# Decayed linear attention in front of two gated layers: the attention's blocks cut from 128 to 64 tokens, its products on quarters of the array

## What is computed

```python
def _attn_ref(q, k, v, alpha):            # (4, 8, 768, 48) each
    B, H, S, D = q.shape
    state = np.zeros((B, H, D, D)); y = np.zeros_like(q)
    for t in range(S):
        state = alpha[:, :, t, :, None] * state + np.einsum('bhd,bhe->bhde', k[:, :, t], v[:, :, t])
        y[:, :, t] = np.einsum('bhd,bhde->bhe', q[:, :, t], state)
    return y

def reference(**kwargs):
    x = attention output as (3072 tokens, 384)
    x = (sigmoid(x @ w_gate) * (x @ w_val)) @ moe_w_out              # 384 -> 1536 -> 384
    return np.maximum(np.maximum(x @ w1, x @ w2), x @ w3) @ w_out    # 384 -> 768 -> 384
...
```

## Time and profile before

| | |
|---|---|
| median of 3 runs | 860.12 us (859.79 to 860.45) |
| the profiled execution, its own time | 859.93 us |
| its span, first to last instruction | 857.9 us |
| PE busy | 851.0 us, 99% |
| DVE busy | 364.2 us, 42% |
| ACT busy | 279.2 us, 33% |
| POOL busy | 75.9 us, 9% |
| chain of work that ended last | PE 97%, DVE 2% |
| mean granted TensorE clock | 0.999 |

### The profile page before, as it was taken

How to read it: one execution, slowest core, us unless ns; L and a number is a source line. 1 busy time by engine, 2 the same in 40 slices (tenths; PEclk the granted TensorE clock), 3 DMA queues, 4 the chain that set the end, 5 groups by cost and what they waited for, 6 DMA issues and landing times.

```text
span 857.9 us, 14194 instructions
## 1 busy us (share of the span) xinstructions
PE 851.0 (99%) x5653; PEld 790.4 (92%) x5653; DVE 364.2 (42%) x677; ACT 279.2 (33%) x520; POOL 75.9 (9%) x68
## 2 busy tenths in 40 slices
PE   8999999999999999999999999999999999999998
PEld 8899999999999999999999999988888888888887
DVE  8776554544454354374265232322323232232321
ACT  4555343333333333333333334421213122131312
POOL 1000111111021021021011004400000000000000
PEclk9999999999999999999999999999999999999999
DMA  7440210210210210201111023100100101010001
GB/s 282 171 169 3 99 47 2 100 47 2 99 47 2 99 47 2 87 17 44 49 51 47 7 74 112 37 1 1 37 1 1 37 0 37 0 37 0 20 17 38
DMA packets 14449, 42.14 MB, mean 49 GB/s; under 512 B 1984, under 2 KB 5952, under 8 KB 14400
## 3 DMA queue, kind: packets, MB, share of 16 engines
q1 hardware_dynamic: 14336, 41.38, 13.5%
q10 hardware_dynamic: 64, 0.05, 0.0%
HBM read 35.52 MB, written 4.72 MB: 47 GB/s over the span
## 4 chain that ended last, share of the span: by engine, by line
PE 97%; DVE 2%; issue 0%; ACT 0%; DMA 0%; ACTq 0%; DVEq 0%
PE ps_gv L915 35%; PE ps_out L940 18%; PE ps_gv L921 17%; PE ps_out L1034 6%; PE ps_sc L915 6%; PE ps_sc L921 3%; PE ps_pair L903 3%; PE ps_sc L866 2%; PE ps_pair L1034 2%; PE ps_pair L850 1%; PE ps_pair L899 1%; PE ps_sc L876 1%; DVE decay L629 0%; DVE rdec L641 0%; DMA inbuf<-att_in 0%
## 5 line engine op out<-in xcount | busy, mean ns | idle before, releaser
L915 PE MATMUL ps_gv<-x_hi,w_hi 128*128 128x384 f32 (+1 forms) x792 | 279.6, 353 | 1.1 <-ACT x_hi L404 1.1
L915 PE MATMUL ps_gv<-x_hi,w_lo 128*128 128x384 f32 (+1 forms) x792 | 277.1, 350 | 0.0
L921 PE MATMUL ps_gv<-x_lo,w_hi 128*128 128x384 f32 (+1 forms) x792 | 234.8, 350 | 0.0
L915 PEld LDWEIGHTS ps_gv<-x_hi,w_hi 128*128 128x128 f32 x792 | 148.7, 188 | 9.3 <-ACT w_hi L404 1.3
L915 PEld LDWEIGHTS ps_gv<-x_hi,w_lo 128*128 128x128 f32 x792 | 148.9, 188 | 7.5
L921 PEld LDWEIGHTS ps_gv<-x_lo,w_hi 128*128 128x128 f32 x792 | 146.0, 188 | 9.4
L719 DVE TENSOR_TENSOR h_sb<-act_sb,ps_gv 128x384 f32<-128x384 f32 x96 | 53.0, 552 | 164.1 <-PE ps_gv L921 163.5
L404 ACT ACTIVATE h_hi<-h_sb 128x384 fp32r<-128x384 f32 x96 | 50.4, 525 | 150.7 <-DVE h_sb L719 150.6
L450 ACT ACTIVATE act_sb<-ps_gv 128x384 f32<-128x384 f32 x96 | 47.2, 491 | 131.2 <-PE ps_gv L921 131.2
L816 DVE TENSOR_TENSOR probs<-probs,ps_gv 128x512 f32<-128x512 f32 x36 | 24.8, 689 | 137.9 <-PE ps_gv L921 137.9
L677 DVE TENSOR_TENSOR h_lo<-h_sb,h_hi 128x384 fp32r<-128x384 f32 x96 | 54.1, 564 | 52.0 <-ACT h_hi L404 52.0
(11 more groups left out here) (123 smaller groups left out, 973.7 us busy)
## 6 DMA issues: line engine op xcount, KB each, us to landing
inbuf<-att_in SPq DMA_DIRECT2D x23, 704.0 KB, 4.7
mid<-w SPq DMA_DIRECT2D x12, 576.0 KB, 8.4
inbuf<-att_in SPq DMA_DIRECT2D x23, 256.0 KB, 3.0
inbuf<-w SPq DMA_DIRECT2D x6, 768.0 KB, 4.3
out<-inbuf SPq DMA_DIRECT2D x5, 768.0 KB, 3.5
x_raw<-x_raw SPq DMA_DIRECT2D x46, 24.0 KB, 1.9
out<-inbuf SPq DMA_DIRECT2D x4, 192.0 KB, 2.0
mid<-att_in SPq DMA_DIRECT2D x1, 704.0 KB, 9.0
```

The source lines that it names most:

```text
L915: mm(bank, w_at(half, f, c + k * P, total=total), x_hi[:, k, 0:w], start=(k == 0 and half == 0), stop=False)
L921: return mm(bank, w_at(0, f, c + k * P, total=total), x_lo[:, k, 0:w], start=False, stop=(k == KT - 1))
```

## The change

Each chunk of 128 tokens is computed as two blocks of `SB` = 64 (`SUBS` = 2).
- `scans` and `recips` make eight scans of 64 and of 63 elements a chunk instead of four of 128 and of 127; a block's decay starts anew.
- `scores` computes only the two diagonal blocks: 16 matmuls, each 48 rows by 64 weight columns with 64 moving columns, on four quarters of the array. `masked` then handles 256 instead of 512 elements a partition, twice. `probs` has two buffers, by the chunk's parity.
- `outer` makes one outer product for each block: 16 matmuls with 64 rows, into two PSUM banks (`ps_sc`, `ps_sc_odd`). It comes ahead of `attend`: after the value product of f = 2, 5, 8.
- `new_state` makes two steps of two VectorE operations instead of one step of two, on three state buffers; it moves from the block after `attend` to f = 2, 5, 8, behind `h_rest`.
- `attend` uses for each block the state ahead of it: 16 matmuls with 64 moving columns (8 where the chunk opens a batch, none before). The values are 16 matmuls of 64 rows and 64 moving columns in two groups of 8; ahead of the second group PE waits for its own semaphore `y_same`, which the last of the first group sets.
- `attend` now waits for this chunk's own new states; in the prologue for the first of the two. `new_state` waits for the `attend` of the chunk before (`y_done`).
- the number of `unused` matmuls in the prologue is changed, and w1's block 5 no longer waits for chunk 1's `probs`, which have moved out of its slot.

```diff
+SB = 64
+SUBS = CH // SB
...
-        probs = sb("probs", [P, H, CH])
-        state = sb("state", [P, 2, PAIRS, D])
+        probs = sb("probs", [P, 2, H, SB])
+        state = sb("state", [P, 3, PAIRS, D])
...
                 for p in range(PAIRS):
-                    nc.vector.tensor_tensor_scan(decay[0:PR, par, p, :], att(buf(Cs), ALPHA)[:, p, :],
-                                                 zero[0:PR, :].broadcast_to([PR, CH]), 1.0, ALU.mult, ALU.add).then_inc(scan_done, 1)
+                    for s in range(SUBS):
+                        nc.vector.tensor_tensor_scan(decay[0:PR, par, p, sub(s)], att(buf(Cs), ALPHA)[:, p, sub(s)],
+                                                     zero[0:PR, :].broadcast_to([PR, SB]), 1.0,
+                                                     ALU.mult, ALU.add).then_inc(scan_done, 1)
...
             def new_state(Cs, i):
 
-                C, cur, new = Cs + 6 * i, Cs % 2, (Cs + 1) % 2
+                C = Cs + 6 * i
                 dve.wait_ge(u_done, C + 1)
...
+                if not (isinstance(i, int) and Cs == 0):
+                    dve.wait_ge(y_done, C)
+                for s in range(SUBS):
+                    next_state(Cs, i, s)
...
-                    done = (C0 + c - 1, i) if att_next and f % 3 == 0 and c > 0 else None
...
-                    if done:
-                        new_state(*done)
+                    if att and f % 3 == 2:
+                        new_state(*att)
...
-                    for r, bank in zip(HALVES, score_banks(Cs, i)):
-                        ins = mm(bank[:, p * CH:(p + 1) * CH], att(buf(Cs), K, r)[:, p, :],
-                                 att(buf(Cs), Q, r)[:, p, :], start=True, stop=True)
+                    for s in range(SUBS):
+                        for r, bank in zip(HALVES, score_banks(Cs, i)):
+                            ins = mm(bank[sub(s), p * SB:(p + 1) * SB], att(buf(Cs), K, r)[:, p, sub(s)],
+                                     att(buf(Cs), Q, r)[:, p, sub(s)], start=True, stop=True)
...
                 for p in range(PAIRS):
-                    for n, r in enumerate(HALVES):
-                        ins = mm(outer_bank(Cs, i)[r, p * D:(p + 1) * D],
-                                 khs[:, p * PR + r.start:p * PR + r.stop],
-                                 v_cols(buf(Cs), (2 * p + n) * D, D), start=True, stop=True)
+                    for s in range(SUBS):
+                        for n, r in enumerate(HALVES):
+                            ins = mm(outer_bank(Cs, i, s)[r, p * D:(p + 1) * D],
+                                     khs[sub(s), p * PR + r.start:p * PR + r.stop],
+                                     v_cols(buf(Cs), (2 * p + n) * D, D)[sub(s), :], start=True, stop=True)
...
+            def value(Cs, i, p, n, s):
+                return mm(y_slot(Cs, i, p, n, s), v_cols(buf(Cs), (2 * p + n) * D, D)[sub(s), :],
+                          probs[sub(s), Cs % 2, PAIRS * n + p, :], start=False, stop=True, skip_group_check=True)
...
+                for s in range(1 if first else 0, SUBS):
                     for p in range(PAIRS):
                         for n, r in enumerate(HALVES):
...
                 for p in range(PAIRS):
                     for n in range(2):
+                        ins = value(Cs, i, p, n, n)
+                ins.then_inc(y_same, 1)
+                pe.wait_ge(y_same, C + 1)
+                for p in range(PAIRS):
+                    for n in range(2):
+                        ins = value(Cs, i, p, n, 1 - n)
                 ins.then_inc(y_done, 1)
...
+                    if att_next and f in (2, 5, 8):
+                        outer(C0 + (f - 2) // 3, i)
                     if att_next and f in (3, 6, 9):
                         attend(C0 + (f - 3) // 3, i)
-                        outer(C0 + (f - 3) // 3, i)
```

More of the change, by code:

```diff
@@ L183, in score_banks, with sub, ends @@
             return ps_sc, ps_sc_odd
[L185 to L189, removed]
+        def sub(s):
+            return slice(s * SB, (s + 1) * SB)
+        def ends(x):
+            return x.rearrange("q a (s t) -> q a s t", s=SUBS)[:, :, :, SB - 1]
         def arrived(eng, sems, Cs, i):
@@ L413, in khs_copy @@
                 act.wait_ge(u_done, C)
-                copy(khs[:, :], u_bank(Cs, i)[:, 0:PAIRS * PR]).then_inc(khs_done, 1)
+                copy(khs[:, :], tr_bank(Cs, i)[:, 0:PAIRS * PR]).then_inc(khs_done, 1)
             def y_copy(Cs, i):
@@ L648, in masked @@
                 if half == 0 and not (isinstance(i, int) and Cs < 2):
[L649 to L652, removed]
+                    dve.wait_ge(y_done, C - 1)
@@ new lines, in new_state, with next_state @@
+                for s in range(SUBS):
+                    next_state(Cs, i, s)
+            def next_state(Cs, i, s):
+                j = Cs * SUBS + s
+                old, new = state[0:PR, j % 3], state[0:PR, (j + 1) % 3]
+                u = outer_bank(Cs, i, s)[0:PR, :].rearrange("p (a e) -> p a e", a=PAIRS)
+                end = decay[0:PR, Cs % 2, :, (s + 1) * SB - 1:(s + 1) * SB].broadcast_to([PR, PAIRS, D])
+                if j % (2 * CPT * SUBS) == 0:
+                    nc.vector.tensor_tensor(new, u, end, ALU.mult).then_inc(state_done, 1)
+                else:
+                    dve.wait_ge(state_done, j + 6 * SUBS * i)
+                    nc.vector.tensor_tensor(stmp[0:PR], u, old, ALU.add).then_inc(stmp_done, 1)
+                    later = j - j // (2 * CPT * SUBS) - 1 + (6 * SUBS - 1) * i
@@ L667, in new_state @@
                     dve.wait_ge(stmp_done, later + 1)
-                    nc.vector.tensor_tensor(state[0:PR, new], stmp[0:PR], end, ALU.mult).then_inc(state_done, 1)
+                    nc.vector.tensor_tensor(new, stmp[0:PR], end, ALU.mult).then_inc(state_done, 1)
             def x_rest(k, n, src, w=TOK):
@@ L891, in attend @@
                     pe.wait_ge(y_evac, C)
[L892 to L896, removed]
+                    pe.wait_ge(state_done, (C + 1) * SUBS)
+                else:
+                    if Cs == 2:
+                        pe.wait_ge(y_evac, 1)
+                    pe.wait_ge(state_done, C * SUBS + 1)
+                for s in range(1 if first else 0, SUBS):
                     for p in range(PAIRS):
                         for n, r in enumerate(HALVES):
-                            mm(y_slot(Cs, i, p, n), state[r, par, p, :], att(buf(Cs), Q, r)[:, p, :],
-                               start=(p < 2), stop=False, skip_group_check=True)
+                            mm(y_slot(Cs, i, p, n, s), state[r, (Cs * SUBS + s) % 3, p, :],
+                               att(buf(Cs), Q, r)[:, p, sub(s)], start=(p < 2 and s == (1 if first else 0)),
+                               stop=False, skip_group_check=True)
                 for p in range(PAIRS):
                     for n in range(2):
-                        ins = mm(y_slot(Cs, i, p, n), v_cols(buf(Cs), (2 * p + n) * D, D),
-                                 probs_of(Cs, i)[:, PAIRS * n + p, :],
-                                 start=(first and p < 2), stop=True, skip_group_check=True)
+                        ins = value(Cs, i, p, n, n)
[4 more added lines that the diff above has]
+                        ins = value(Cs, i, p, n, 1 - n)
                 ins.then_inc(y_done, 1)
@@ L989, in general, with unused @@
                     ins.then_inc(gen_sum, 1)
-            def unused(n, left, right):
+            def unused(n, bank, left, right):
                 for _ in range(n):
-                    mm(ps_out[:, 2, 0:CH], left, right, start=True, stop=True)
+                    mm(ps_out[:, bank, 0:right.shape[-1]], left, right, start=True, stop=True)
             zeros = state[:, 0, :, :].rearrange("p a e -> p (a e)")
             pe.wait_ge(state_zero, 1)
-            unused(15, zeros[:, 0:P], zeros[:, D:D + CH])
+            unused(12, 2, zeros[:, 0:P], zeros)
             scores(0, 0)
@@ L1007, in _ @@
             attend(0, 0)
+            unused(4, 0, ident, ident)
             outer(1, 0)
-            unused(10, ident, mask)
+            unused(7, 0, ident, ident)
             scores(2, 0)
```

87 lines of the change are left out of this document (46 added, 41 removed).

## The result

The changed kernel takes **863.1 us** (median of 7 runs, 861.54 to 863.53) against 860.43 (859.79 to 860.72) of the kernel before in the same session: ratio 1.0029, interval 1.002 to 1.0039. It is slower by 0.3%, where 856.9 and "faster" were forecast, and lies 0.1 us above the range.

A forecast was written before the change was run, and what follows sets the result against it. PE's instruction stream was taken as the bound (busy 851.0 of 857.9 us). Layer 1 -6.7 and prologue +3.5 sum to -3.2: 856.7 on the profiled run, 856.9 us as median; range 851.8 to 863.

The forecast's parts named there:

- the prologue's chain: Prologue: scores of chunk 2 start once its k is scaled, 2.3 us later; copy of y and first product +3.5 us.
- The `unused` matmuls fill PE's waits and don't shift this: Prologue: the filler matmuls on PE add nothing to the +3.5 us delay of the first product.
- Rival 2: Prologue takes the gain: half scans cost nearly a whole, or longer chain, +6 and more; `y_same` dearer; 860 to 862, chance 0.2.
- Its clause on longer waits at half clock: Prologue: longer PE waits ahead of the first product could cost a stretch at half clock; part of the 0.2 chance.
- the groups of four at 0.058: PE inside layer 1: a group of four passes with 64 columns takes 0.058 us, interpolated between 0.046 and 0.108.
- `attend` 1.55 (1.57): PE inside layer 1: state and value matmuls with the wait on `y_same` sum to 1.57 us a chunk.
- a batch-opening chunk at 0 (-0.48 + 0.46): Layer 1, three chunks: scores save 0.48 us, outer and attend add 0.46, since half a state product is new.
- layer 1 -6.76 (-6.7): PE over layer 1's 21 chunks: scores -10.1, outer and attend +2.0 and +1.4, together -6.7 us.
- h's delay covered: VectorE inside layer 1: h comes 1.0 us late but costs nothing, with 4.7 us of PE work as cover.
- forecast +0.7: Prologue, VectorE: half scans, forward and backward, take 0.7 us more a chunk, between 0 and +3.0.
- Rival 1: PE in layer 1: too many passes, averaging no less than 0.023 us; +24 us, 881 us; chance 0.13 in full or part.
- The test that the prediction set: Prologue: a first product after 33 us would show the forecast wrong; near 31.2 would show it right.

The follow-up runs named there:

- the first experiment: The changed kernel, but outer(1) in the prologue waits for chunk 0's masks alone, not chunk 1's; 857.56 us, ratio 0.9971.
- the fifth experiment: The kernel of the first experiment with chunk 1's two states made ahead of chunk 2's masks on VectorE; 857.6 us, ratio 0.9965.
- second experiment: The changed kernel with 22 instead of 4 unused matmuls between attend(0) and outer(1) in the prologue; 860.83 us, ratio 1.0008.

## Why the prediction was wrong

**The failed step** is the prologue's chain: "PE's scores of chunk 2 start when chunk 2's k is scaled", and its sum +3.5. It followed the scores to their own releaser and not to what stands ahead of them on PE. The change gives `outer` a wait that it did not have, on `mask_done` (the two lines taken out in the first experiment; the cut diff ahead of the prediction leaves them out); inside layer 1 the masks are long done, and no outer product waited there, and the same line in the prologue went unpriced. The measured sum is +7.55. Taking that one wait away gives +3.39 and 857.56 us, 0.7 over the forecast, so nothing else of size is missing.

**"The `unused` matmuls fill PE's waits and don't shift this"** failed with it. That holds while they end ahead of the releaser. Behind a late `outer(1)` at half clock, seven of them held the scores back by 2.8 us.

**Rival 2** had the side and nearly the size (860 to 862; 863.1 measured) but mostly not the mechanism: neither half scans nor `y_same` were dearer than reckoned. Its clause on longer waits at half clock came true and is worth 2.0 to 2.3 us.

**Right:** the groups of four at 0.058; scores 1.18 (1.16); outer 0.72 (0.71); `attend` 1.55 (1.57); a batch-opening chunk at 0 (-0.48 + 0.46); layer 1 -6.76 (-6.7); no wait on another engine in front of `outer` or `attend` inside layer 1; h's delay covered. Eight half scans took 1.57 (1.37 for four whole in the earlier trace rows) and the backward ones 2.03 (1.60): +0.63 a chunk, forecast +0.7.

**Rival 1** and the rule of the Trainium skill beside it ("TensorEngine Tiling (Array Packing)", Instruction Overhead) did not bind: four passes in 0.058 us leave each quarter more than the page's 60 cycles (an estimate of 25 ns at 2.4 GHz), but each pass only 0.0145 us on average, so the rule doesn't hold for the row of passes.

**The test that the prediction set** ("a first product after 33") is met at 35.27.

**Open:** the 0.55 us hole in the fifth experiment; and how much of the 0.8 us in the last output's landing belongs to the change, since nothing ahead of it differs. From the start of the last PE pass to the end of the span it is 3.31 us before, 4.10 in the changed kernel and 4.10 to 5.06 in the seven experiments, one execution each: the landing varies by a microsecond among kernels that don't differ there.

## What to carry to other kernels

When a change gives a helper a new wait, follow it at every place where the helper is called, the prologue too, and ask what is queued ahead of the signal on the other engine; a wait that costs nothing in the steady loop cost 5.2 to 5.5 us once here, most of the 6.76 that the 21 chunks of layer 1 gave. A wait for a late-ordered signal can often name an earlier one that protects the same buffer. And PE's stand of 4.1 us cost its length and then 3.2 us of work at half clock; the filler inside the wait (second experiment) gave the clock's part back, while the seven `unused` behind it delayed the chain. So filler belongs into the wait, sized to end just ahead of the releaser.

## What the runs showed of the hardware

- PE waiting on its own semaphore costs 0.30 us a time. A second such wait made a chunk's state and values 1.65 us instead of 1.34, and the kernel 7.0 to 7.2 us longer for 24 of them; at both places the last pass ahead of the wait and the first behind it start 0.30 us apart.
- Four passes on four quarters with 64 columns start 0.058 us apart as a group, against 0.108 for 128 columns.
- The granted clock fell to 0.51 behind a stand of 4.09 us, and in one execution to 0.54 after waits of 1.26 and 1.08 us, while others of the same kernel show a mean of 1.0.
- A scan of 64 columns takes 0.20 us in the prologue (1.57/8), one of 128 takes 0.34 (1.37/4): at one slope, 0.05 is fixed (an estimate from these two).
